# Turning attention probabilities by VectorE squares and summing them in four row groups

## The reference, cut to what matters

```python
# q, k, v: (2, 8, 768, 64), 16 heads of 768 rows; all fp32
mask = q_bucket[:, :, :, None] == k_bucket[:, :, None, :]   # 6 sign bits of q @ proj, k @ proj
scores = scale * np.matmul(q, k.transpose(0, 1, 3, 2))
scores = np.where(mask, scores, -1000000000.0)
scores = scores - np.max(scores, axis=-1, keepdims=True)
attn = np.exp(scores)
attn = attn / (np.sum(attn, axis=-1, keepdims=True) + 1e-09)
out = np.matmul(attn, v)
# then: logits = x @ w_gate, experts chosen in order of the logits, each expert relu(x @ w1) @ w2,
# then silu(h) @ w_out with h = x @ w_in
```

## Time and profile before

| | |
|---|---|
| median of 3 runs | 818.46 us (816.99 to 820.39) |
| profiled execution | 819.84 us, span 817.9 us, mean granted TensorE clock 0.992 |
| TensorE busy | 795.9 us, 97% |
| VectorE busy | 513.9 us, 63% |
| ScalarE busy | 272.1 us, 33% |
| GpSimd busy | 100.1 us, 12% |

### The profile page before, as it was taken

How to read it: one execution, slowest core, us unless ns; L and a number is a source line. 1 busy time by engine, 2 the same in 40 slices (tenths; PEclk the granted TensorE clock), 3 DMA queues, 4 the chain that set the end, 5 groups by cost and what they waited for, 6 DMA issues and landing times.

```text
span 817.9 us, 14884 instructions
## 1 busy us (share of the span) xinstructions
PE 795.9 (97%) x5566; PEld 642.7 (79%) x5572; DVE 513.9 (63%) x1217; ACT 272.1 (33%) x586; POOL 100.1 (12%) x137
## 2 busy tenths in 40 slices
PE   8899999999999988999999999999999999999996
PEld 5667666666666645999999999998888788878885
DVE  6888888888888697888779773173332433243231
ACT  4566666666666621212212212221012111121101
POOL 4101221312123301011011100000000100010001
PEclk9999999999999989999999999999999999999999
DMA  5141624425141104344546338720000100010001
GB/s 117 40 102 21 139 58 86 96 45 131 44 107 55 36 21 168 138 173 136 201 130 206 136 129 300 262 103 0 1 1 5 46 0 0 0 51 0 0 0 52
DMA packets 73035, 68.27 MB, mean 83 GB/s; under 512 B 50752, under 2 KB 58944, under 8 KB 71968
## 3 DMA queue, kind: packets, MB, share of 16 engines
q1 hardware_dynamic: 69440, 60.43, 24.6%
q0 software_dynamic: 2208, 7.21, 2.7%
q10 hardware_dynamic: 1344, 0.04, 0.1%
HBM read 61.38 MB, written 6.29 MB: 83 GB/s over the span
## 4 chain that ended last, share of the span: by engine, by line
PE 91%; DVE 4%; issue 1%; DMA 1%; ACT 1%; POOL 1%; ACTq 0%; DVEq 0%; POOLq 0%
PE pt_ps L1501 16%; PE score_ps L1484 15%; PE pt_ps L1390 10%; PE pt_ps L1402 10%; PE pt_ps L1272 8%; PE pv_ps L1220 5%; PE score_ps L1208 4%; PE score_ps L1220 4%; PE score_ps L1209 4%; PE work_ps L1332 2%; PE score_ps L1181 1%; PE work_ps L1181 1%; DMA area<-x_rows,ids_now 1%; PE pt_ps L1229 1%; PE score_ps L1378 1%
## 5 line engine op out<-in xcount | busy, mean ns | idle before, releaser
L1501 PE MATMUL pt_ps<-y_s,w_in_s 128*128 128x512 f32 x576 | 137.8, 390 | 2.7 <-DVE y_s L1136 2.0
L1484 PE MATMUL score_ps<-w_out_s,gate_s 128*128 128x512 f32 x576 | 137.4, 389 | 0.0
L1501 PEld LDWEIGHTS pt_ps<-y_s,w_in_s 128*128 128x128 f32 x576 | 107.9, 188 | 26.1 <-DVE y_s L1136 2.8
L1484 PEld LDWEIGHTS score_ps<-w_out_s,gate_s 128*128 128x128 f32 x576 | 108.2, 188 | 22.4
L1154 DVE TENSOR_TENSOR gate<-pt_ps,sig 128x512 f32<-128x512 f32 x48 | 33.2, 692 | 146.3 <-ACT sig L648 146.3
L514 ACT ACTIVATE att_area<-att_area 128x768 f32<-128x768 f32 x96 | 90.0, 937 | 89.7 <-DVE att_area L852 89.7
L852 DVE TENSOR_SCALAR_CACHE_REDUCE att_area<-score_ps 128x768 f32<-128x768 f32 x96 | 91.8, 956 | 21.1 <-PE score_ps L1209 19.7
L1390 PE MATMUL pt_ps<-area,experts_w 128*128 128x192 f32 x512 | 97.6, 338 | 1.5 <-ACT area L608 1.2
L648 ACT ACTIVATE sig<-pt_ps 128x512 f32<-128x512 f32 x48 | 28.7, 598 | 210.5 <-PE pt_ps L1501 210.5
L1402 PE MATMUL pt_ps<-area,experts_w 128*128 128x192 f32 x512 | 87.2, 328 | 0.0
L1390 PEld LDWEIGHTS pt_ps<-area,experts_w 128*128 128x128 f32 x512 | 83.1, 192 | 2.1 <-ACT area L608 2.1
(11 more groups left out here) (208 smaller groups left out, 1025.2 us busy)
## 6 DMA issues: line engine op xcount, KB each, us to landing
experts_w<-in_moe_w SPq DMA_DIRECT2D x16, 2048.0 KB, 8.4
experts_w<-in_k SPq DMA_DIRECT2D x15, 384.0 KB, 4.4
experts_w<-in_q SPq DMA_DIRECT2D x15, 384.0 KB, 5.2
experts_w<-in_moe_w_in SPq DMA_DIRECT2D x8, 512.0 KB, 4.9
w_out_raw<-in_moe_w_out SPq DMA_DIRECT2D x4, 1024.0 KB, 8.1
att_area<-in_v SPq DMA_DIRECT2D x16, 192.0 KB, 2.4
x_rows<-att_area SPq DMA_DIRECT2D x8, 384.0 KB, 3.1
area<-x_rows,ids_now POOLq DMA_INDIRECT x16, 4.0
```

What stands on the lines that cost most here:

```text
L1484: done = nc.tensor.matmul(out_ps[m], gate_s[:, fo % RING_S, a, m * P:(m + 1) * P], w_out_s[:, fo, b, :], start=(fo == 0 and a + b == 0), s ...
L1501: done = nc.tensor.matmul(layer_ps[f % 2][:, 0:GT], w_in_s[:, a, w_cols], y_s[:, c, b, :], start=(c == 0 and a + b == 0), stop=(c == DC - ...
```

## The change

The turned probabilities are laid out in squares of Q = 32. VectorE turns a whole tile of 128 x 768 with one `transpose`, each 32 x 32 square in its place: after it, partition group a (32 partitions) of column block b holds the probabilities of query rows 32a to 32a + 31 against keys of block b. The copies of `pt_ps` by VectorE and ScalarE and the transposes on TensorE are gone. The weighted sum then contracts over 32 partitions at a time: for each of KB = 24 key blocks and each of four row groups one product, 64 columns of v as weights and 6 x 32 = 192 streamed columns. Row group a writes to PSUM bank a of `quad_ps`; even key blocks go to partitions 0 to 63, odd ones to 64 to 127, and the two sums are added in "x" (`to_x` now has the identity twice, one under the other, and `w_gate` twice). So that every row group has v on its own partitions, v is loaded four times, 32 partitions each (`v_quarters`).

The weighted sum's blocks are dealt to the tiles of the next head by `SHARE = [0, 6, 6, 8, 0, 4]`. `quad_ps` takes four banks and is one for all heads, so the weighted sum of a head waits until that of the head before is copied (`s_turned`). The second preparation bank is now `pv_ps`. The minimum of tile n + 2 also waits until the transpose that read the same `probs` buffer is done. "x" has six products of 72 columns instead of three of 144.

```diff
-            def turned(h, p):
+            def turned(h):
                 act.wait_ge(s_pv, h + 1)
-                nc.scalar.activation(weighted_t[p], pv_banks[p][:, 0:HALF], ACT.Copy).then_inc(s_turned, 1)
+                nc.scalar.activation(weighted_t.rearrange("p (t a j) -> p a t j", t=T, j=Q), sums_ps, ACT.Copy).then_inc(s_turned, 1)
...
             def load_v(h, p):
-                sp.dma_start(v_nat[p], head(v_rows, h)).then_inc(s_v[p], 16)
+                src = v_rows[bass.ds(h, 1)].rearrange("a i m n -> i (a m) n")
+                for a in range(P // Q):
+                    sp.dma_start(v_quarters[p][Q * a:Q * (a + 1)], src).then_inc(s_v[p], 16)
...
-                        act.wait_ge(s_pt[1], n + 1)
-                        nc.scalar.activation(probs_t[p][t // TH][:, TH:T, t % TH, :],
-                                             pt_ps[1][:, 0:HALF].rearrange("p (a b) -> p a b", a=3), ACT.Copy).then_inc(s_ptc[1], 1)
...
             def max_tile(n, c):
                 dve.wait_ge(s_scores, n + 1)
+                if not (isinstance(n, int) and n < 3):
+                    dve.wait_ge(s_pt, n - 2)
...
-                        dve.wait_ge(s_pt[0], n + 1)
+                        dve.wait_ge(s_exp, n + 1)
                         if t == 0 and not first:
                             dve.wait_ge(s_pv, h - 1)
-                        nc.vector.tensor_copy(probs_t[p][t // TH][:, 0:TH, t % TH, :],
-                                              pt_ps[0][:, 0:HALF].rearrange("p (a b) -> p a b", a=3)).then_inc(s_ptc[0], 1)
+                        nc.vector.transpose(probs_t[p][:, t, :], probs[c % 3]).then_inc(s_pt, 1)
...
-            def weighted(h, p, b, loads):
-                if b == 0:
-                    for part in range(2):
-                        pe.wait_ge(s_ptc[part], T * h + T)
-                    pe.wait_ge(s_v[p], 16 * loads + 16)
-                for half in range(2):
-                    done = nc.tensor.matmul(pv_banks[p][half * D:(half + 1) * D, 0:HALF], v_nat[p][:, b, :],
-                                            probs_t[p][half][:, b, :, :].rearrange("p t q -> p (t q)"),
-                                            start=(b == 0), stop=(b == T - 1))
+            def weighted(h, p, b0, n, loads):
+                if n and b0 == 0:
+                    pe.wait_ge(s_pt, T * h + T)
+                    pe.wait_ge(s_v[p], 64 * loads + 64)
+                    pe.wait_ge(s_turned, h)
+                for b in range(b0, b0 + n):
+                    for a in range(P // Q):
+                        rows = slice(Q * a, Q * (a + 1))
+                        side = slice(D * (b % 2), D * (b % 2 + 1))
+                        done = nc.tensor.matmul(quad_ps[side, 512 * a:512 * a + QT],
+                                                v_quarters[p][rows, b % 4, D * (b // 4):D * (b // 4 + 1)],
+                                                probs_t[p][rows, :, Q * b:Q * (b + 1)], start=(b < 2), stop=(b >= KB - 2))
...
-                        pe.wait_ge(s_exp, n + 1)
-                        for half in range(2):
-                            if not (first and c == 0):
-                                pe.wait_ge(s_ptc[half], n)
-                            for b in range(3):
-                                done = nc.tensor.transpose(pt_ps[half][:, b * P:(b + 1) * P],
-                                                           probs[c % 3][:, (3 * half + b) * P:(3 * half + b + 1) * P], ident[:, :])
-                            done.then_inc(s_pt[half], 1)
...
-                            weighted(h - 1, 1 - p, t, g if p else g - 1)
+                            weighted(h - 1, 1 - p, sum(SHARE[0:t]), SHARE[t], g if p else g - 1)
```

More of the change, by code:

```diff
@@ L50, in routed_layers @@
     HALF = 3 * P
-    DE = 2 * (D + E)
+    DE = D + E
+    Q = 32
+    KB = S // Q
     TH = T // 2
@@ L182, in routed_layers @@
         x_nat = att(T, P)
[L183 to L187, removed]
         head_logits = att(T, E)
@@ L191, in routed_layers @@
         row_inv = att(2 * T)
-        probs_t = [[att(T, HALF) for _ in range(2)], [expert_w(4 * T * P + s * T * HALF, 0, T * HALF).rearrange("p (b n) -> p b n", b=T) for s in range(2)]]
-        probs_t = [[half.rearrange("p b (t q) -> p b t q", t=TH) for half in head] for head in probs_t]
-        assert 4 * T * P + 2 * T * HALF <= W1 + W2
+        bit_proj = att(P)
+        to_x = att(H, DE)
+        v_quarters = [att(P // Q, T * D) for _ in range(2)]
+        probs = [att(S) for _ in range(3)]
+        weighted_t = att(S)
+        probs_t = [att(T, S), expert_w(4 * T * P, 0, T * S).rearrange("p (t n) -> p t n", t=T)]
+        assert 4 * T * P + T * S <= W1 + W2
         used[0] = DC * N
@@ L249, in routed_layers @@
         s_exp = sem("probs_ready")
-        s_pt = [sem(f"probs_transposed{i}") for i in range(2)]
-        s_ptc = [sem(f"probs_copied{i}") for i in range(2)]
+        s_pt = sem("probs_turned")
         s_pv = sem("pv_ready")
@@ L526, in _ @@
             exp_tile(1, 1)
-            act.wait_ge(s_gate_zero, 1)
-            for i, r0 in enumerate((0, D)):
-                act.dma_start(to_x[r0:r0 + D, :, P + E * i:P + E * (i + 1)], w_gate.rearrange("(h d) e -> d h e", d=D)).then_inc(s_wg, 16)
+            for r0 in (0, D):
+                act.dma_start(to_x[r0:r0 + D, :, D:DE], w_gate.rearrange("(h d) e -> d h e", d=D)).then_inc(s_wg, 16)
             def first_batch_row_out(c):
@@ L692, in more_constants @@
                 step(nc.gpsimd.memset(pending[:, :], 1.0))
-                step(nc.gpsimd.tensor_copy(to_x[:, :, 0:P], ident[:, :].unsqueeze(1).broadcast_to([P, H, P])))
+                for r0 in (0, D):
+                    rows = slice(r0, r0 + D)
+                    step(nc.gpsimd.tensor_copy(to_x[rows, :, 0:D], ident[rows, rows].unsqueeze(1).broadcast_to([D, H, D])))
                 step(nc.gpsimd.memset(assigned[:, :, :], 0.0))
@@ L1192, in fill_work @@
                     pe.wait_ge(s_turned, h + 1)
-                    for t in range(TH):
-                        last = nc.tensor.matmul(bank[:, t * DE:(t + 1) * DE], weighted_t[p_next][:, t * P:(t + 1) * P], rhs,
+                    for t in range(T):
+                        last = nc.tensor.matmul(bank[:, t * DE:(t + 1) * DE], weighted_t[:, t * P:(t + 1) * P], rhs,
                                                 start=True, stop=True)
@@ L1232, in _ @@
             pe.wait_ge(s_ones, 1)
[L1233 removed]
+            keep_busy(13, idle_bank)
             pe.wait_ge(s_const, 1)
@@ L1297, in _ @@
             pair(PAIRS - 1, False, True)
-            for b in range(T):
-                weighted(HEADS - 1, 1, b, PAIRS - 1)
-                if b == 1:
-                    fill_work("x", 0, W_LAST - 1, HEADS - 2, 0, 0, work_banks[0])
+            weighted(HEADS - 1, 1, 0, 8, PAIRS - 1)
+            fill_work("x", 0, W_LAST - 1, HEADS - 2, 0, 0, work_banks[0])
+            weighted(HEADS - 1, 1, 8, KB - 8, PAIRS - 1)
             fill_work("x", 0, W_LAST, HEADS - 1, 1, 0, work_banks[1])
```

50 lines of the change are left out of this document (23 added, 27 removed).

## The result

The changed kernel takes 828.26 us (median of 4 runs, 827.25 to 828.48), the kernel before 817.73 (4 runs, 816.55 to 820.39): a ratio of 1.0122, 95% interval 1.0094 to 1.0149. It is 1.2% slower. Predicted were 825 us, 6.5 more than the 818.46 then known; measured are 828.26, 10.5 more than the kernel before.

A forecast was written before the change was run, and what follows sets the result against it. TensorE was taken to bound the kernel at 17.36 us a head, VectorE afterwards at 17.72. Heads 0 to 2 +2.9, heads 3 to 14 +4.3, head 15 -0.5: +6.7, so 825 us; range 797 to 858.

The forecast's parts named there:

- A: The forecast itself: VectorE is the new bound in the attention stage; 825 us, own range 817 to 836, chance 0.57.
- The transpose: VectorE's new transpose of a 768-column tile, taken as 0.96 us at one column a cycle.
- B: Rival: VectorE's transpose runs at the pace of a one-source SBUF pass, 0.61 us; 801 us, chance 0.19.
- E: Rival: VectorE's transpose takes two cycles a column, 1.76 us; about 900 us, chance 0.06.
- The sum of a head: VectorE's work summed over a head's six tiles, from one minimum to the next: 17.72 us, against 17.36 before.
- TensorE's need: TensorE per head: 8.1 us stays, 5 for new products, 0.9 for shape changes; 14 us, no longer the bound.
- C: Rival: the weighted sum's row groups overlap only in part, priced at three at a time; 857 us, chance 0.12.
- D: Rival: only two weighted-sum products in flight on TensorE, as before; 940 us, chance 0.06.
- Heads 0 to 2: First three heads: VectorE's sums give 52.0 us for 49.10, +2.9.
- Head 15 and the end: Last head gains 0.5 us from shorter intervals; the stretch after it nets 0.
- The clock: TensorE's granted clock falling to its lower level, a sign against the forecast: about 28 us a head; no case set.
- The loads of v: v read as four copies, 768 KB for 192 KB: stays hidden; uncovered it would cost about 2.4 us a head.

The follow-up runs named there:

- e8: Changed kernel plus four dummy TensorE products of 512 columns in each of the first five tiles of head 0; 827.07 us.
- e7: Changed kernel with VectorE's k_bits and q_bits drains moved: ScalarE takes signs, GpSimd makes bits by multiply-add; 811.93 us, ratio 0.9928 to the kernel before.
- e5: Changed kernel with all 96 products of a head reading partitions 0 to 31, so one row group and two places instead of eight; 1309.6 us.
- e9: Changed kernel with all key blocks except block 1 summing into partitions 0 to 63, so four places instead of eight; 847.86 us.
- e7b: As e7, with squares dealt [0, 4, 6, 6, 4, 4] and dummy TensorE products in head 0; 810.59 us, ratio 0.9918 to the kernel before.
- e11: As e7b, with squares dealt [5, 6, 0, 4, 4, 5] and VectorE's pairs 1 to 6 written out; 807.33 us, ratio 0.9864 to the kernel before.

## Why the prediction was right, step by step

**The bound moves to VectorE.** Shown by the half transpose (-22 us), the half products (no gain) and the doubled copy in the old kernel (+18 us). Two of the signs named for A came out otherwise in size: TensorE is busy 85% of the stretch and not 80, VectorE 94% and not 99. The eight shown matmuls that run together start within 0.05 us, as said.

**The transpose.** 0.96 us was taken, 0.977 measured over 96. The estimate from the Trainium skill ("VectorE: DVE Perf Modes", The three transpose paths) was 978 ns; by that, the trace agrees. The half one took 0.577, so (977 - 577) / 384 = 1.04 ns a column and 0.18 us beside, nearly the line of the earlier trace rows. Rivals B and E are out.

**The sum of a head.** Predicted 17.72, measured 17.83. The terms in their order: 3.40 against 3.08 and 3.66 by turns (mean 3.37: I had put a fraction of the loop's turn into each head, and it is 0.58 us in every second one); 3.17 against 3.17; 3.17 against 3.19; 3.29 against 3.32; 2.03 against 2.03; 2.66 against 2.77. The last holds a wait of 0.32 us for x that the sum did not have; the rest of it was a little shorter than summed.

**TensorE's need.** 5 + 0.9 us a head was taken for the new products; blocks of 1.16, 1.16, 1.48 and 0.83 make 4.6. With TensorE busy 15.2 us a head it had over 2 us to spare, as said. The eight places run fully side by side (0.162 / 8 = 20 ns), so rivals C and D are out.

**Sizes that were off.** Heads 0 to 2 lost 4.3 us, not 2.9. VectorE's own sums left out a wait: the scores of head 1 wait for its bits, whose last drain now stands behind a transpose, and TensorE, idle for 2.75 us before, then runs them at its lower clock (about 0.7 us of it, by e8):

```profile
28.72 0.76 PE L1206 MATMUL score_ps<-k_high,q_parts 128*128 128x512 f32 x1 [2.75 <-DVE q_bits L822]
```

Head 15 and the end gained 1.9, not 0.5. In head 15, with fewer drains, the shorter loop shows (1.1). Behind the last minimum it is 0.9, but there the kernel before also had the lower clock for 10.2 us and the changed one for 3.4; the two causes were not separated. The errors at the two ends nearly cancel, which is luck; heads 3 to 14 gave 5.6 for 4.3. Sum +7.6 of span for +6.7.

The medians lie 10.5 us apart, not 7.6. The profiled execution of the changed kernel (827.25) was the fastest of its four, that of the kernel before (819.84) is above its median of 817.73. So about 3 us of the difference are in no row of the traces. The prices of B, C and D in the prediction start from the profiled 819.84 and that of A from the median, 1.4 less.

**The clock.** I had named its fall as a sign that would prove the forecast wrong. In the changed kernel's heads 3 to 14 it fell for 3.4 us three times and cost nothing, because VectorE set the pace; below are two heads with the same loop turn, at 0.91 and at 1.00. Where TensorE is close to the pace it does cost: about 0.7 us at the end of head 0, 1.1 us each time in e7, 1.3 us once in e8, and in e5 it is a main part of the time. The prediction had no price for a partial fall.

```profile
82.97:101.15 18.18, 15.85 (x251) 12.10 (x250) 16.71 (x30) 8.50 (x18) 5.55 (x6) 0.91 0.77 170
...
154.42:172.56 18.14, 15.02 (x251) 11.13 (x249) 16.71 (x30) 8.51 (x18) 5.56 (x6) 1.00 0.78 173
```

**The loads of v.** Four of them, landing after 4.0 us instead of 2.4, with the DMA share at 0.49 instead of 0.33: hidden, as no wait in the attention names them; it was not tried by itself.

## What to carry to other kernels

Before work is moved from a full engine to one with 17% to spare, sum the receiving engine's instructions between two marks of the period, not its busy share: 0.4 us more for each of six tiles was all it took to lose what the relief of TensorE could have bought (9 us of work taken off a head, 4.6 put on in its place). Sum it interval by interval too, for every engine: a mean over the head hides the one tile where another engine holds (e9, e7), and after each repair the bound was a different one. The change paid only once its receiver was unloaded, and then by 1.4%. The same unloading of the kernel before was not tried; there TensorE had no idle time in these heads. And before a small gain is put down to an edit, look at the granted clock of both runs (e7b).

## What the runs showed of the hardware

- Products of 32 rows by 64 columns in eight different places of TensorE ran all together: 20 ns a shown matmul of 192 fp32 columns, 41 ns in the four row groups of one column half. In one row group, the two column halves ran side by side: 0.168 us each in the middle of a block at the lower clock, 0.088 at the full one, and 0.190 over a whole block at the lower clock, because at its ends one place worked alone (e5).
- TensorE's granted clock was 0.59 in a stretch where the engine was busy all the time, mostly with such products in two places (e5). A busy engine is not by itself one at full clock.
- GpSimd's compare over 768 columns took 2.78 to 2.85 us for 32 or 64 partitions; its multiply-add over 64 partitions 0.91.
- ScalarE's Sign between exponentials came without a table load, at the 0.49 us of a copy.
- The turn of VectorE's hardware loop cost 0.58 us on the path, six times, and 2.8 us came back when it was written out (e11).
- VectorE's fp32 transpose in squares of 32 took 1.04 ns a column and 0.18 us beside (977 ns for 768 columns, 577 for 384).
